# One weight matrix for two Gram products, a first power padded by VectorE, and an MLP that normalises between its factors

## The reference, cut to what matters

```
for t in range(S):                                  # S = 768, B = 4, H = 8 heads, D = 40
    y[t]  = r[t] . state
    Sa    = state . a[t]
    state = state * w[t] - outer(Sa, b[t]) + outer(v[t], k[t])
x = moe_attention(y)                                # 4 experts, causal softmax, top 2
h = relu(x @ w_in); u, v = halves of h              # 512 columns each
v_n = (v - mean(v)) / sqrt(var(v) + 1e-6)
out = (u * (w_spatial @ v_n + b_spatial)) @ w_out
```

## Time and profile before

| what | value |
|---|---|
| median of 3 runs | 1017.11 us (1008.78 to 1019.47) |
| the profiled execution, its own time | 1006.58 us |
| its span in the trace | 1004.7 us |
| PE busy | 956.4 us (95%) |
| DVE / ACT / POOL busy | 521.8 / 462.3 / 238.7 us |
| recurrence, first L898 to the last beat's end | about 30 to 482 us |
| mean granted TensorE clock | 0.991 of full speed |

### The profile page before, as it was taken

One profiled execution on the slowest core, in us unless ns is written; L12 is line 12 of the kernel. 1 busy time (PEld: TensorE's weight loads), 2 busy tenths in 40 slices (PEclk: granted clock), 3 DMA queues, 4 the chain that ended last, 5 costly groups with the idle time before them and its releaser, 6 DMA issues.

```text
span 1004.7 us, 36936 instructions
## 1 busy us (share of the span) xinstructions
PE 956.4 (95%) x15708; PEld 687.9 (68%) x15708; DVE 521.8 (52%) x1443; ACT 462.3 (46%) x1122; POOL 238.7 (24%) x344
## 2 busy tenths in 40 slices
PE   6799999999999999989998999999999999999898
PEld 4678888888888888876646655676556665567455
DVE  7677777787787777654344244312443124431210
ACT  6455655665655655643247334443344333343401
POOL 7344444354354444311000001100011000110011
PEclk8899999999999999999999999999999999999999
DMA  4244434354334334251150100001000000000001
GB/s 147 73 112 115 122 106 132 98 153 119 103 97 127 102 100 123 70 140 30 40 175 1 40 0 1 1 34 47 1 1 1 34 8 1 1 1 34 8 1 39
DMA packets 51539, 63.68 MB, mean 63 GB/s; under 512 B 27440, under 2 KB 37488, under 8 KB 51376
## 3 DMA queue, kind: packets, MB, share of 16 engines
q1 hardware_dynamic: 51376, 61.32, 20.8%
HBM read 53.42 MB, written 7.86 MB: 61 GB/s over the span
## 4 chain that ended last, share of the span: by engine, by line
PE 81%; DVE 11%; issue 5%; ACT 3%; DMA 1%; DVEq 0%; ACTq 0%
PE banks L1627 13%; PE banks L662 7%; PE banks L726 6%; PE banks L1567 5%; PE banks L1545 4%; PE banks L1519 4%; PE banks L1596 4%; PE banks L1639 4%; PE banks L1609 4%; PE banks L1579 4%; DVE state_z L1140 4%; PE banks L908 3%; PE banks L898 3%; PE banks L773 3%; PE banks L657 2%
## 5 line engine op out<-in xcount | busy, mean ns | idle before, releaser
L510 ACT ACTIVATE powers_z<-powers,parity 128x256 f32<-128x256 f32 x240 | 108.9, 502 | 165.7 <-DVE powers L1013 165.6
L1390 POOL TENSOR_TENSOR v_st<-v_st,u_t 128x384 f32<-128x384 f32 x32 | 31.9, 998 | 478.5 <-DVE v_st L1779 478.5
L1627 PE MATMUL banks<-w_st,v_n 128*128 128x384 f32 x384 | 140.4, 501 | 4.9 <-issue 4.9
L726 PE MATMUL banks<-pq,powers_z 64*64 64x64 f32 (+1 forms) x3072 | 133.1, 224 | 11.5 <-issue 6.0
L726 PEld LDWEIGHTS banks<-pq,powers_z 64*64 64x64 f32 x3072 | 112.0, 137 | 18.2 <-issue 7.8
L458 POOL TENSOR_TENSOR state<-state_sum,dc 128x160 f32<-128x160 f32 x92 | 68.8, 748 | 175.5 <-DVE state_sum L1126 175.5
L1395 ACT ACTIVATE probs_t<-banks 128x512 f32<-128x512 f32 (+1 forms) x96 | 51.9, 543 | 120.8 <-PE banks L1567 120.7
L1627 PEld LDWEIGHTS banks<-w_st,v_n 128*128 128x128 f32 x384 | 68.3, 192 | 53.5 <-issue 17.4
L1118 DVE SCALAR_TENSOR_TENSOR vu_tok<-banks,minus,vz_tok 128x80 f32<-128x80 f32 x192 | 48.8, 296 | 70.2 <-PE banks L908 70.2
L1725 DVE CUSTOM_DVE_ANT_0 probs<-banks,hide 128x128 f32<-128x128 f32 (+5 forms) x96 | 56.0, 622 | 51.8 <-PE banks L1545 51.4
L1409 ACT ACTIVATE probs<-probs,neg_max 128x128 f32<-128x128 f32 (+5 forms) x96 | 63.5, 662 | 31.3 <-DVE neg_max L1725 31.3
(11 more groups left out here) (165 smaller groups left out, 1809.0 us busy)
## 6 DMA issues: line engine op xcount, KB each, us to landing
w_all<-decays_dram SPq DMA_DIRECT2D x48, 160.0 KB
w_all<-kb_ch_dram SPq DMA_DIRECT2D x48, 160.0 KB
vz_tok<-vz_tok_dram SPq DMA_DIRECT2D x24, 320.0 KB, 3.6
r_all<-rz_ch_dram SPq DMA_DIRECT2D x48, 160.0 KB
x_dram<-y_tok SPq DMA_DIRECT2D x384, 10.0 KB, 2.0
a_raw<-a_ch_dram SPq DMA_DIRECT2D x48, 80.0 KB
vc_tok<-vc_tok_dram SPq DMA_DIRECT2D x24, 160.0 KB, 4.2
r_all<-r_ch_dram SPq DMA_DIRECT2D x48, 80.0 KB
```

What stands on the lines that cost most here:

```text
L510: act.activation(powers_z[:, i, :, j, :], powers[:, i, :, :], ACT.Copy, scale=parity[:, j:j + 1])\
L726: ins = pe.matmul(to[r, k * n:k * n + n], powers_z[r, i, k, :, :].rearrange("p j t -> p (j t)"), right, start=True, stop=True)
L1627: ins = pe.matmul(bank[M_BANK + j % 2][:, 0:TH], v_n[:, i, d * P:d * P + P], w_st[:, i, t], start=(i == 0), stop=(i == BLOCKS - 1))
```

## The change

In the recurrence, `grams` is called once for a unit, in step (0, 0). Each of its 16 matmuls takes 64 columns of weights (32 of keys and 32 of b, which lie side by side in `kb_ch`) and writes 64 partitions, so bank 6 is filled by one pass, and both kinds are interleaved there. DVE masks the whole 512 columns twice: with `straight` into `n_z` (N, already padded) and with `crossed` into `akz`. It transposes all of `n_z` straight into `powers_z`, so ACT's two copies for level 0 are gone. N without padding, `n_t`, is now the sum of the two halves of `n_z`, made by POOL ahead of `first_factor`'s addition. Level 0 moves: its first half from (1, 1) to (2, 1), its second from (2, 1) to behind level 3 in (2, 2); level 2 is split 4 and 4 instead of 2 and 6. In the MLP, DVE does the variance after factor piece 4, the inverse deviation after piece 5 and block 0 of the normalisation after piece 6; matmul i of the first dense group waits for block i alone.

```diff
@@ POOL, constants
+            pool.memset(straight[:, :, :], 0.0).then_inc(consts, 1)
...
-                pool.tensor_copy(upper[r, 0:2, :], square[r, :, r]).then_inc(consts, 1)
+                pool.tensor_copy(upper[r, :], square[r, 1, r]).then_inc(consts, 1)
+                pool.tensor_copy(straight[r, g % 2, :], square[r, 0, r]).then_inc(consts, 1)
@@ POOL, first_factor
                 pool.wait_ge(n_read, at(u, n_read))
+                if u > 0:
+                    pool.wait_ge(level_ready[0], at(u - 1, level_ready[0]))
+                pool.tensor_tensor(n_t[:, :, :], n_z[:, :, 0, :], n_z[:, :, 1, :], ALU.add).then_inc(n_joined, 1)
+                pool.wait_ge(n_joined, at(u, n_joined))
@@ ACT
-                if valid(t):
-                    spread_power(t, 0)
@@ PE, grams
+                to = bank[GRAM_BANK].rearrange("p (c x j t) -> p c x j t", x=2, j=2, t=C)
                 for c in range(NC):
                     for q in range(Q):
                         a, p, g, blk = place(c, q)
-                        slot = 1 - a if kind == 0 else a
-                        col = (kind * NC + c) * 2 * C
-                        ins = pe.matmul(bank[GRAM_BANK][rows32(2 * p + slot), col:col + 2 * C],
-                                        kb[:, (a * NC + c) * 2 + p, slot, :],
+                        first = (a * NC + c) * P + p * 2 * C
+                        ins = pe.matmul(to[rows64(p), c, :, 1 - a, :], kb_ch[:, u % 3, first:first + 2 * C],
                                         az_ch[:, blk, :, :], start=True, stop=True)
@@ PE, level
-                    pe.wait_ge(spread[i], at(u, spread[i]))
+                    if i == 0:
+                        pe.wait_ge(turned[0], at(u, turned[0]))
+                        pe.wait_ge(n_joined, at(u, n_joined))
+                        pe.wait_ge(akz_read, at(u, akz_read))
+                    else:
+                        pe.wait_ge(spread[i], at(u, spread[i]))
@@ PE, between
                 if (c, j) == (1, 1):
-                    if valid(t):
-                        level(t, 0, 0, 4)
                     if valid(v):
-                        level(v, 2, 0, 2)
+                        level(v, 2, 0, 4)
                 if (c, j) == (1, 2) and valid(v):
-                    level(v, 2, 2, N8)
+                    level(v, 2, 4, N8)
                 if (c, j) == (2, 0):
-                    if valid(t):
-                        grams(t, 1)
...
                 if (c, j) == (2, 1):
                     if valid(t):
-                        pe.wait_ge(akz_read, at(t, akz_read))
-                        level(t, 0, 4, N8)
+                        level(t, 0, 0, 4)
                     if valid(v):
                         level(v, 3, 0, 2)
-                if (c, j) == (2, 2) and valid(v):
-                    level(v, 3, 2, N8)
+                if (c, j) == (2, 2):
+                    if valid(v):
+                        level(v, 3, 2, N8)
+                    if valid(t):
+                        level(t, 0, 4, N8)
@@ DVE, first_power and keys_of_a
+            def from_grams(u, dst, mask):
+
+                every = [P, N8, 2, C]
+                return dve.tensor_tensor(dst, bank[GRAM_BANK].rearrange("p (k j t) -> p k j t", j=2, t=C),
+                                         mask[:, :, :].unsqueeze(1).to_broadcast(every), ALU.mult)
...
-                turn_power(u, 0, n_t[:, :, :])
+                dve.transpose(powers_z[:, 0].rearrange("p k j t -> p (k j) t"),
+                              n_z[:, :, :, :].rearrange("p k j t -> p (k j) t")).then_inc(turned[0], 1)
@@ PE, dense
                         if x == 0:
                             pe.wait_ge(w_late, W_LATE)
-                            pe.wait_ge(v_normed, at(m, v_normed, BLOCKS))
+                        if j == 0:
+                            pe.wait_ge(v_normed, at(m, v_normed, i + 1))
@@ DVE, MLP
+                        if j == 2 * DT - 4:
+                            variance(m)
+                        if j == 2 * DT - 3:
+                            inverse_deviation(m)
+                        if j == 2 * DT - 2:
+                            normalise(0)
-                    inverse_deviation(m)
-                    for i in range(BLOCKS):
+                    for i in range(1, BLOCKS):
                         normalise(i)
```

69 lines of the change are left out of this document (29 added, 40 removed).

## The result

The changed kernel takes 1024.43 us (median of 4 runs, 1021.09 to 1028.10); the kernel before took 1013.49 on the same chip (median of 4, 1008.78 to 1019.47). The ratio is 1.0105, with a 95% interval from 1.0054 to 1.0155. The forecast was 1029.6, from 1013 to 1037. The profiled execution of the changed kernel took 1022.67 us, with a span of 1020.9 and a mean granted clock of 0.982 (before: 1006.58, 1004.7 and 0.991).

The account below looks back on a forecast made before the run. PE's work was taken to bound steps j = 0, a latency chain the rest of each chunk. Recurrence +15.4, start +1.5 and MLP -4.4 gave +12.5 us, added to the 1017.11 median: 1029.6 us, range 1013 to 1037.

Parts of the forecast that it names:

- Chunk 0: First of a beat's four chunks: Gram products +0.52, DVE's instructions +0.54, `state_z` -0.30, in sum +0.76 us.
- DVE's term: Chunk 0, between `vu_tok` and `state_sum`: mask +0.27, transpose +0.27, `state_sum` 0.54 us later; `state_z` 0.30 shorter.
- The Grams' term: Wide Gram products make step (0, 0) 0.52 us longer and their removal makes (2, 0) 0.56 shorter.
- Chunk 1: Second chunk of a beat: level 0's first half leaves slack places, POOL's joining addition fits its idle time: 0.
- Chunk 2: Third chunk: Gram products leave, but the wait for ACT's copy and moved level 0 matmuls remain: -0.06 us.
- level 0 stays hidden: Rival: in chunk 2 DVE's chain sets the end at 4.8; +6.1 us in all, 1023.2; chance 0.20.
- Half as many matmuls therefore cost the same: Gram products: 16 wide matmuls take 1.08 us, the two narrow kinds 2 x 0.56 = 1.12.
- The start: Level 0 of unit 0 waits for POOL's joining addition, to 15.7 instead of 14.28: +1.5 us.
- The MLP: Last sequence: PE's 4.91 us of idle time ahead of dense mostly goes, -4.4 us.
- The lock and the transpose: Rival: transpose doubles, and `state_z` keeps 0.79 or the join blocks DVE's scan; +0.48 a beat, 1040.2; chance 0.10.
- faster: Rival: longer Gram products slip under a wait at chunk 0's L908, chunk 2 gains whole; -9.9 us, 1007.2; chance 0.08.
- the edits cancel: Rival: copy wait and transpose not as sized, beat within 0.2 us, total within 5 us of before, 1017; chance 0.12.

Follow-up runs that it names:

- e2_mask_early: The changed kernel with DVE's mask and transpose of the first power moved into step (0, 0), ahead of `vu_tok`: 1021.9 us in one run.
- e4_half_level0: The changed kernel without the second half of level 0 for units 2 and up, its done signal one step earlier; output not the reference's: 1003.94 us in one run.
- e1: The kernel before with the MLP part of the change alone: 1007.06 us, ratio 0.9917.
- e3: The changed kernel with POOL's first factor of unit 0, joining addition included, ahead of the keys of unit 1: 1019.3 us in one run.
- e8: The kernel before with the recurrence part of the change alone, the MLP as before: 1025.41 us, ratio 1.0119.
- e5: The changed kernel with each 64-column Gram matmul made as two of 32 columns, in the same place: 1023.39 us in one run.
- e6: The kernel before with the new MLP, and the second Gram products moved from step (2, 0) to (0, 2): 1008.84 us, ratio 0.9926.
- e7: The kernel before with the new MLP, second Gram products moved to step (0, 2) and level 3 whole in (2, 2): 1007.73 us, ratio 0.9917.
- e9: The changed kernel with narrow Gram products, DVE's mask and transpose early, and the join of unit 0 ahead of unit 1's keys: 1020.11 us, ratio 1.0105.
- e11: The changed kernel with wide Gram products kept, DVE's mask and transpose early, and the join ahead of unit 1's keys: 1012.72 us, ratio 0.9965.
- mended recurrence: The changed recurrence with early mask and transpose and the join first, with narrow (e9, ratio 1.0105) or wide (e11, 0.9965) Gram products.

## Why the prediction was right, and where it was not

The direction, the place and the mechanism were right: slower, by chunk 0, while step (2, 0) keeps almost nothing of what it gave up. By spans the recurrence's twenty beats cost +13.1 against 14.0 predicted. That closeness is partly luck: errors cancel in it, and it hangs on which two executions are compared.

**Chunk 0**: +0.86 measured, +0.76 predicted. DVE's term is exact: `state_sum` 0.54 later, the transpose 0.71 (0.72), `state_z` back to 0.49. What hides behind that 0.30 is a second limit: in the twelve beats of before in which chunk 0 takes 4.82 to 4.84, `state_z` lasts anything from 0.50 to 0.80 us and yet ends at 4.77 each time, 0.35 behind the end of POOL's `kb_ch`. So up to 0.3 us of delay in DVE's queue cost nothing there, and the Grams, the mask and the transpose paid only for what went beyond. The Grams' term was too small: L913 comes 2.57 after L903 instead of the 2.47 that I named, since the wide Grams start 0.11 later behind the 32-column state products than narrow ones, and the sum took only their duration. e2_mask_early shows DVE's part (0.60) to be real and avoidable.

**Chunk 1**: 4.20, as predicted. The join stands in POOL's gap.

**Chunk 2**: +0.02 measured, -0.06 predicted. L913 comes 2.22 after L903, where I had 2.10: L669 starts 0.28 after L903 there, and the narrow Grams that stood before it started at 0.16. It is the same 0.1 as in chunk 0, of following 32-column matmuls. The wait for ACT's copy is there as described: level 3 starts 3.24 after L903 (3.20 predicted), 0.14 behind the copy's end, and moves with it in units 11 and 21. e4_half_level0 confirms the floor of the rival "level 0 stays hidden" at 4.83 and shows that the eight matmuls cost 0.35: that rival was wrong for the reason given.

**"Half as many matmuls therefore cost the same"** is the weakest step. It holds for the undisturbed beat and not for the kernel. Beats take more than their medians: 9.9 us over twenty beats before, 5.2 after, while the undisturbed beat rose by 0.89. So 17.8 - 4.7 = 13.1. The Grams' term had no gain for waits on issue. Counted over the beats, they are 8.3 and 9.7 us with the recurrence of before (before and e1) and 2.3 to 4.3 with the changed one (after, e3 and e8); narrow Grams in the changed kernel bring them back to 10.8 (e5). So the term left out a gain of some 4 to 8 us. Nor is +13.1 a firm number: e1_mlp_alone has the recurrence of before, and its twenty beats took 380.2 us, 5.5 more than those of the trace of before. Against it the three traces of the changed beats (385.8 to 388.3) cost 5.6 to 8.1 us.

**Units 0 and 1** have no term of their own in the sum; they stood in 22 x 0.70 with 1.4 us and cost 4.65. e4_half_level0 shows that nearly all of it comes with the moved half of level 0.

**The start**: +1.76 against +1.5, and level 0 starts at 16.22 (15.7 or later). Only the second is sure. Three kernels with the old start (e1_mlp_alone, e6 and e7) have their first state products at 32.14, 31.49 and 31.48, where the profiled execution of before had 29.81. By these four and the five with the new start, the old one is 1.0 us shorter. The join first, as in e3, e9 and e11, gives 1.2 us back, so the join's place on POOL is the term's cause, as predicted.

**The MLP**: -6.4 against -4.4. The idle time went as predicted. What was left out is what followed it: behind the 4.91 us of idle time the clock was at half. Granted clock of before from 956 to 960 us:

```profile
956.00:960.00 4.00, 4.00 (x8) 2.12 (x9) 0.00 (x0) 0.00 (x0) 0.00 (x0) 0.57 0.00 0
```

and timeline of DVE before, its first two reads of dense groups:

```profile
961.80 0.56 DVE L1779 TENSOR_TENSOR v_st<-banks,bias 128x384 f32<-128x384 f32 x1 [5.94 <-PE banks L1627]
965.67 0.56 DVE L1779 TENSOR_TENSOR v_st<-banks,bias 128x384 f32<-128x384 f32 x1 [3.31 <-PE banks L1627]
```

The first group of six matmuls took 961.80 - 955.96 = 5.84 us, the second 3.87. In the changed kernel the second matmul starts after 0.16 of idle time and the clock stays full (1.00 from 973.6 to 985 us). The Trainium skill ("TensorE: Matmul & The Clock Gate", Part 1) describes a clock that is halved after idleness, and the rows agree: 1.2 GHz behind the gap, 2.4 GHz where there is none. The mis-sized term is the -4.4, by 1.6 to 2 us. The prediction had this cost before it and read it away: it took the merged row, 14 records in 6.45 us, for ten matmuls with records missing. None is missing (the page before counts 384 for L1627, two for each of 192 matmuls). The 14 records are seven matmuls, at 0.92 us each, and not ten at 0.65.

**The attention of sequence 0** took 2.5 us more in the one profiled execution, with half clock from 537 to 544 us. e2_mask_early has it too; e8_recurrence_alone, e3_join_first and e11_wide_mended, with the same recurrence, don't. It does not belong to the change in every execution, and I leave its cause open.

**The rivals.** The lock and the transpose did not cost their most (0.49 and 0.71). The stated range (1013 to 1037) left out the times of two of the rivals, 1040.2 and 1007.2. Nothing hid the longer Grams at L913 of chunk 0, so "faster" fell at the place where it was to be decided, and with a beat 0.9 longer "the edits cancel" fell too.

**The level.** The difference of the medians measured on one chip is +10.9, of the spans +16.2, predicted +12.5. The profiled execution of before had a higher clock (0.991) than most of its runs, so the spans differ by more than the medians. The forecast's 1029.6 is 5.2 too high; 3.6 of that is the median to which I added, 1017.11 of three runs, where a fourth run made it 1013.49.

## What to carry to other kernels

In a loop that is a chain of latencies on in-order engines, price an edit by its place: an instruction between two links costs its full time (0.60 us of an undisturbed chunk for a mask and a transpose there, nothing one step earlier), and work that leaves a stretch is replaced by the next wait behind it. Then look at what the undisturbed beat doesn't show: compare the sum of many beats with their median, read "issue" in the view of PE's waits and hold it against the landings of PE's instruction packets, and prefer fewer, wider matmuls in such a loop even where their pitch says that they are worth the same. And take the gap and what the clock does behind it as one term.

The best version found is the kernel before with the new MLP alone (0.9917); e7_level3_late has the same ratio, and no mended recurrence beat it.
